# Wider token groups in a fused attention, FFN and expert kernel: 384 tokens for 256, and both halves of a pair's output in one go

## The chip, the cores and the metric

One core of one Trainium2 chip. The metric is the device time of one execution in microseconds (us), as the median of several runs. The kernel is written in Bass: each of the five engines (PE the matmul engine, DVE, ACT, POOL, SP) has its own list of instructions in a fixed order, and engines wait for one another through counting semaphores.

## The reference

Three stages follow one another. A linear attention with decay (4 batches, 8 heads, 768 steps, head size 48) gives `x` of 3072 tokens by 384. A gated layer without a nonlinearity then computes `h = ((x @ w1) * (x @ w2)) @ w3 @ w_out`, with an inner width of 1024. At last a noisy top-2 routing sends each token to two of eight experts, each a pair of matrices 384 by 1024 and 1024 by 384 with a ReLU between, and adds the two weighted results:

```python
for t in range(S):
    cur = np.einsum('bhd,bhe->bhde', u[None] * kt, vt)
    y[:, :, t] = np.einsum('bhd,bhde->bhe', rt, state + cur)
    state = wt[:, :, :, None] * state + np.einsum('bhd,bhe->bhde', kt, vt)
...
h = a * b @ w3
return (h @ w_out).astype(np.float32)
...
noisy_logits = logits + noise_scale * noise
top2 = np.argpartition(-noisy_logits, 2, axis=1)[:, :2]
...
h = np.maximum(x[mask] @ w1[e], 0.0)
out[mask] += top2_w[mask, k, None] * (h @ w2[e])
```

## The kernel before, in words

Every product is made from three matmuls of rounded parts (high by high, high by low, low by high), in a float type that PE runs at one column a cycle.

The program has three parts in time. **First part** (to about 107 us): the attention of batch 0, and beside it `w3 @ w_out` with the gate columns folded in (`wah`, `wal`, 400 columns wide), and the split of `w1` and `w2` into parts (`w12h`, `w12l`). **Middle part**: for batches 0 to 2, the gated layer works through the tokens of batch b in groups of TG = 256 (NG = 3 groups a batch) while the attention of batch b+1 is threaded between, pair of heads by pair of heads (HP = 4 pairs). **Finale**: the groups of batch 3 alone, then 31 visits of experts (4 early, 27 late), each of which gathers 256 or 128 token rows, multiplies them by an expert's matrices and adds the result into `result`.

A group runs through these steps. `turn`: ACT and DVE split the group's tokens, which SP has loaded from DRAM into a buffer (`xr`, three of them), into `xh` and `xl`. `up`: for each of eight blocks f of the inner width PE makes a and b side by side in one bank of PSUM (`pe_up`, line 807, 18 matmuls of 256 columns), ACT copies a out (`act_up`, L852), DVE multiplies it by b (`dve_up`, L885), ACT rounds the product (L848), DVE takes the rest (L878). Two banks alternate, so block f waits until block f-2 is multiplied. `down`: for each 128 tokens (ST = 2 tiles) 24 matmuls of 400 columns (`pe_down`, L823) into `fx` or bank 1; ACT copies the sum to `x2s` (L863), and SP stores 384 of its columns to DRAM (`sp_group_store`, L787). `route`: some twenty small operations of DVE and three of ACT choose two experts for each token. `place`: PE makes running counts (L836, L838), DVE turns them into slots, and POOL scatters one 8-byte entry for each token and choice into the table `slot_entry` in DRAM (`pool_scatter`, L985): one indirect DMA of 128 entries for each tile and choice, 4 for a group. `place` of a group comes in the `down` of the next one, after its first tile. `dve_place` waits at L967 until all scatters before its own have landed.

In the attention each pair of heads has steps too: `in` (transposes, L162), `score` (L177, into `pp`), `keys` (L186), `state` (L198), `scale`, and `out`: `pe_output` (L217 and L223) sums the output of half a batch's steps in the bank `yu`, ACT copies it to `yt` (L354), and the second half waits for that copy before it goes into the same bank.

The order on each engine comes from lists: `group_steps` gives the steps of a batch's groups, `pair_slots` those of the attention, and `threaded` deals the first over ten slots a pair in proportion to LENGTH. For the finale a loop adds the experts' steps by hand. There `split` n casts the n-th of seven pieces of an expert's weights (ACT, L1303, which waits for `piece_loaded`) and takes the rest (DVE, L1308); `tokens` transposes gathered rows (PE, L1199).

SP issues nearly all loads and stores in one order of its own and waits in it. For the first expert visit it waits until the scatters of batches 0 to 2 have landed (L1080), reads the expert's number, loads `who` (L1090) and then the seven pieces (L1100, L1104). POOL gathers rows for a visit (L1117), and the gather of visit 2 stands behind the scatters of the last group in POOL's order.

```python
elif kind == "down" and q == 1 and 1 <= n <= 4:
    finale.append(("split", 0, n - 1))
elif kind == "up" and q == 2 and n in (1, 3, 5):
    finale.append(("split", 0, 4 + n // 2))
elif kind == "down" and q == 2:
    finale.append(("tokens", 0, 0) if n == 0 else ("split", 1, n - 1))
```

## Time and profile before

| | |
|---|---|
| median of 3 runs | 1050.72 us (1050.07 to 1050.78) |
| profiled execution, own time | 1052.72 us |
| its span | 1051.0 us |
| granted TensorE clock, mean of the span | 0.99 |
| busy: PE, weight load, DVE, ACT, POOL | 96%, 91%, 67%, 56%, 21% |
| chain that ended last | PE 86%, DMA 4%, DVE 3%, issue 2% |
| matmul instructions | 7769 |
| first part, middle part with finale's groups, visits | about 0 to 107.7, to 541.8, to 1051 us |

The page is one execution. Busy times of PE hold overlaps: one matmul's record lasts longer than the distance to the next. What a stream of matmuls costs is read from the chain of waits, where a piece gives the time and the number of instructions. Idle time in square brackets stands before an instruction, with what ended it. The clock column is 1.00 at 2.4 GHz and 0.50 at 1.2 GHz.

### The profile page before, as it was taken

The numbers are of one execution on the slowest core, as the hardware profiler recorded it, in microseconds if no ns is written. First come the engines' busy times: TensorE is split into PE (matmuls) and PEld (weight loads), VectorE is DVE, ScalarE is ACT, GpSimd is POOL, SyncE is SP. The second block draws the span as 40 slices with busy tenths as digits, with TensorE's granted clock in tenths as the row PEclk, the third lists the DMA queues.
The fourth block names the chain that finished last, engine by engine and source line by source line (L and its number), as shares of the span: only waits on it lengthen the run. The fifth ranks groups of instructions, "written<-read, shape, count | busy, mean of one in ns | idle before, by whom it ended". The sixth has DMA issues, their size and how long they took to land.

```text
span 1051.0 us, 20538 instructions
## 1 busy us (share of the span) xinstructions
PE 1012.4 (96%) x7769; PEld 952.1 (91%) x7769; DVE 705.0 (67%) x1339; ACT 584.8 (56%) x1126; POOL 218.3 (21%) x210
## 2 busy tenths in 40 slices
PE   6999999989999899999998999999999999999995
PEld 5666899978999899999997999999999999999995
DVE  5887768666788687735685667575765857576570
ACT  4666445536555456533563566575665756566471
POOL 0000000110110110111324232433333234333421
PEclk9999999998999999999999999999999999999998
DMA  9655332333343422130757879787888978788851
GB/s 258 151 155 154 77 80 67 72 89 75 77 93 83 109 55 50 43 73 31 242 129 111 260 202 298 210 256 222 247 251 217 299 210 249 243 227 267 226 158 16
DMA packets 190887, 166.42 MB, mean 158 GB/s; under 512 B 118258, under 2 KB 174452, under 8 KB 190788
## 3 DMA queue, kind: packets, MB, share of 16 engines
q1 hardware_dynamic: 177012, 144.76, 48.2%
q0 software_dynamic: 12976, 20.32, 9.7%
q8 instruction: 62, 1.02, 0.5%
q14 instruction: 37, 0.30, 0.1%
q10 hardware_dynamic: 800, 0.02, 0.0%
HBM read 141.21 MB, written 25.22 MB: 158 GB/s over the span
## 4 chain that ended last, share of the span: by engine, by line
PE 86%; DMA 4%; DVE 3%; issue 2%; another core or an unknown queue 1%; POOL 1%; ACT 1%; SPq 1%; POOLq 0%; DVEq 0%; ACTq 0%
PE bank L807 19%; PE bank L1220 17%; PE pp L1236 17%; PE fx L823 5%; PE bank L823 5%; PE tr L162 3%; PE yu L1279 3%; PE yu L223 2%; PE pp L177 2%; PE fx L699 2%; PE bank L699 2%; PE yu L217 2%; PE tr L1199 2%; DMA xr<-ffn_out,who 2%; PE yu L1261 1%
## 5 line engine op out<-in xcount | busy, mean ns | idle before, releaser
L807 PE MATMUL bank<-xh,w12h 128*128 128x256 f32 x576 | 168.0, 292 | 0.6 <-DVE xl L483 0.6
L807 PE MATMUL bank<-xl,w12h 128*128 128x256 f32 x576 | 163.6, 284 | 0.8 <-issue 0.7
L807 PE MATMUL bank<-xh,w12l 128*128 128x256 f32 x576 | 163.5, 284 | 0.0
L1130 POOL DMA_INDIRECT result<-x2s,who x55 | 92.5, 1681 | 289.7 <-ACT x2s L1353 277.7
L1340 DVE SCALAR_TENSOR_TENSOR abl<-bank,abh 128x512 fp32r<-128x512 f32 x96 | 66.2, 690 | 111.7 <-ACT abh L1335 107.4
L985 POOL DMA_INDIRECT slot_entry<-entry,slot_i x48 | 48.5, 1010 | 381.1 <-DVE token_f L974 369.9
L807 PEld LDWEIGHTS bank<-xh,w12h 128*128 128x128 f32 x576 | 110.9, 193 | 3.3 <-issue 1.4
L807 PEld LDWEIGHTS bank<-xh,w12l 128*128 128x128 f32 x576 | 110.9, 193 | 1.0 <-issue 1.0
L807 PEld LDWEIGHTS bank<-xl,w12h 128*128 128x128 f32 x576 | 111.1, 193 | 0.0
L1220 PE MATMUL bank<-xh,set_up_h 128*128 128x256 f32 x384 | 109.2, 284 | 0.0
L1220 PE MATMUL bank<-xh,set_up_l 128*128 128x256 f32 x384 | 108.6, 283 | 0.0
L1220 PE MATMUL bank<-xl,set_up_h 128*128 128x256 f32 x384 | 108.6, 283 | 0.0
L1335 ACT ACTIVATE abh<-bank 128x512 fp32r<-128x512 f32 x96 | 57.5, 599 | 86.6 <-PE bank L1220 78.9
L885 DVE TENSOR_TENSOR ab_all<-a_sb,bank 128x256 f32<-128x256 f32 x96 | 40.2, 419 | 89.3 <-ACT a_sb L852 78.3
L1236 PE MATMUL pp<-set_down_h,abh 128*128 128x384 f32 x256 | 87.7, 343 | 0.0
L1236 PE MATMUL pp<-set_down_h,abl 128*128 128x384 f32 x256 | 85.7, 335 | 0.0
L1236 PE MATMUL pp<-set_down_l,abh 128*128 128x384 f32 x256 | 85.6, 334 | 0.0
L1117 POOL DMA_INDIRECT xr<-ffn_out,who x55 | 73.1, 1329 | 49.7 <-issue 25.9
L258 DVE RECIPROCAL kdiv<-decay 128x256 f32<-128x256 f32 x48 | 83.0, 1739 | 0.2
L852 ACT COPY a_sb<-bank 128x256 f32<-128x256 f32 x96 | 35.3, 368 | 85.6 <-PE bank L807 76.1
L1353 ACT ACTIVATE x2s<-pp,who 128x384 f32<-128x384 f32 x48 | 28.0, 582 | 84.8 <-PE pp L1236 79.8
L1220 PEld LDWEIGHTS bank<-xh,set_up_h 128*128 128x128 f32 x384 | 73.5, 191 | 0.5 <-DVE abl L1340 0.2
(249 smaller groups left out, 2752.1 us busy)
## 6 DMA issues: line engine op xcount, KB each, us to landing
up_raw<-in_moe_w SPq DMA_DIRECT2D x93, 512.0 KB
down_raw<-in_moe_w SPq DMA_DIRECT2D x124, 384.0 KB
padded<-in_w SPq DMA_DIRECT2D x32, 144.0 KB, 2.8
padded<-in_k SPq DMA_DIRECT2D x32, 144.0 KB, 2.8
padded<-in_r SPq DMA_DIRECT2D x32, 144.0 KB, 2.9
vs<-in_v SPq DMA_DIRECT2D x32, 144.0 KB, 2.9
attention_out<-yt SPq DMA_DIRECT2D x64, 72.0 KB, 1.9
xr<-attention_out SPq DMA_DIRECT2D x12, 384.0 KB, 3.4
```

Of the source, the lines that this page charges most:

```text
L258: nc.vector.reciprocal(kdiv[q % 2][:, :].rearrange("p (c x) -> p c x", c=NC)[:, two, :], decay[q % 2][:, two, 1:C + 1]).then_inc(inverse_r ...
L699: last = nc.tensor.matmul(sums[q % 2][:, 0:WA], w3T[q % 2][:, m, :], wo[:, m, :], start=(m == 0), stop=(m == KF - 1))
L807: last = nc.tensor.matmul(bank[f % 2][:, m * TG:(m + 1) * TG], wp[:, m, kk, f * P:(f + 1) * P], xp[:, kk, :], start=(n == 0), stop=(n == 3 ...
L823: last = nc.tensor.matmul(sum_at[s][:, 0:WA], xp[:, f, s * P:(s + 1) * P], wp[:, f, :], start=(f == 0 and n == 0), stop=(f == KF - 1 and n ...
L885: nc.vector.tensor_tensor(ab[f % 4], a_sb[f % 2][:, :], bank[f % 2][:, TG:2 * TG], ALU.mult).then_inc(ab_free, 1)
L985: nc.gpsimd.indirect_dma_start(slot_entry, bass.IndirectOffsetOnAxis(slot_i[:, s, n:n + 1], 0), entry[:, s, n, :], None).then_inc(scattere ...
L1117: nc.gpsimd.indirect_dma_start(xg[v % 2][:, s, :], None, stored, bass.IndirectOffsetOnAxis(who[v % 4][:, s, 0:1], 0)).then_inc(gathered[v ...
L1130: nc.gpsimd.indirect_dma_start(out, bass.IndirectOffsetOnAxis(who[v % 4][:, s, 0:1], 0), yo[v % 2][:, s, 0:DM], None, bounds_check=N - 1, ...
L1220: last = nc.tensor.matmul(bank[m % 2][:, f * T2:(f + 1) * T2], wp[:, kk, c:c + P], xp[:, kk, :], start=(n == 0), stop=(n == 3 * KD - 1))
L1236: last = nc.tensor.matmul(pp[:, s, 0:DM], xp[:, f, s * P:(s + 1) * P], wp[:, f, :], start=(f == 0 and n == 0), stop=(f == KF - 1 and n == 2))
L1335: nc.scalar.activation(hh[:, 2 * m:2 * m + 2, :].rearrange("p a t -> p (a t)"), bank[m % 2][:, :], ACT.Relu).then_inc(hh_ready, 1)
L1340: nc.vector.scalar_tensor_tensor(hl[:, 2 * m:2 * m + 2, :].rearrange("p a t -> p (a t)"), bank[m % 2][:, :], 0.0, hh[:, 2 * m:2 * m + 2, : ...
```

## The change

TG goes from 256 to 384, so a batch has NG = 2 groups and each group ST = 3 tiles. One block of a or b of 384 columns no longer shares a bank with the other: `up` has 16 steps a group (block f, then m = 0 for a and m = 1 for b), each 9 matmuls of 384 columns, in the three banks `bank[0]`, `bank[1]`, `fx` in turn (`half_bank`). Step n waits for what freed its bank: ACT's copy of a, or DVE's product, of step n-3. The tiles of `down` are summed in bank 1, `fx`, bank 1. A scatter of a group has six indirect DMAs, not four.

To find the memory, the three token buffers become one (`turned_in`, which is loaded again only when the tokens before it are turned), the three `x2s` one (ACT waits at the next `down` for its store), the four product buffers three, and some tables lie in other buffers' memory.

`pe_output`: the state's part of all six chunks is summed first, then the scores' part of half 0, then of half 1, half 0 in `yu` and half 1 in the first bank of `pp`; both `out` steps stand in one slot. PE no longer waits for ACT's copy of half 0, and the next pair's scores wait for both copies.

In the finale, `split` of visit 0 starts in the `up` of the last group (group 1) at its step 4, every second step, and `split` of visit 1 in its `down` from part 3. `store` of the finale's first group moves behind the first visit's loads on SP.

```diff
-TG = 256
+TG = 384
+HALVES = 2
...
-LENGTH = {"up": 8, "down": 6, "turn": 0, "route": 0, "place": 0,
+LENGTH = {"up": 6, "down": 6, "turn": 0, "route": 0, "place": 0,
...
+        def output_bank(half):
+
+            return (yu[:, 0:S // 2], pp[:, 0, 0:S // 2])[half]
+
         def pe_output(pe, b, q, half):
+
             g = HP * b + q
             if half == 0:
-                pe.wait_ge(state_ready, (NC - 1) * g + 2)
-                pe.wait_ge(att_ready, 2 * g + 1)
                 pe.wait_ge(yu_free, g + 1)
-            else:
                 pe.wait_ge(att_ready, 2 * g + 2)
                 pe.wait_ge(state_ready, (NC - 1) * (g + 1))
-                pe.wait_ge(y_ready, 2 * g + 1)
...
-                     [("out", q, 0), ("derive", q + 1, 1)],
-                     [("out", q, 1), ("in", q + 1, 2), ("derive", q + 1, 2)],
+                     [("out", q, 0), ("out", q, 1), ("derive", q + 1, 1)],
+                     [("in", q + 1, 2), ("derive", q + 1, 2)],
...
-                if q < 2:
-                    sp.wait_ge(y_stored[q], 32 * HP * (b + 1))
-                if not (isinstance(b, int) and b == 0):
-                    sp.wait_ge(turn_free, 2 * (NG * (b - 1) + q) + 2)
-                sp.dma_start(tokens_of(q), xa[:, bass.ds(b * S + q * TG, TG)].rearrange("(k p) t -> p k t", p=P)
+                sp.wait_ge(y_stored[q], 32 * HP * (b + 1))
+                need(sp, turn_free, 2 * (NG * b + q))
+                sp.dma_start(turned_in, xa[:, bass.ds(b * S + q * TG, TG)].rearrange("(k p) t -> p k t", p=P)
...
+                elif n >= 3:
+                    pe.wait_ge((a_ready, ab_free)[(n - 3) % HALVES], KF * i + (n - 3) // HALVES + 1)
+                p = 0
+                for kk in range(KD):
+                    for wp, xp in ((w12h, xh), (w12h, xl), (w12l, xh)):
+                        last = nc.tensor.matmul(half_bank[n % 3][:, 0:TG], wp[:, m, kk, f * P:(f + 1) * P], xp[:, kk, :],
+                                                start=(p == 0), stop=(p == 3 * KD - 1))
+                        p += 1
+                last.then_inc((a_full, b_full)[m], 1)
...
-                elif kind == "down" and q == 1 and 1 <= n <= 4:
-                    finale.append(("split", 0, n - 1))
-                elif kind == "up" and q == 2 and n in (1, 3, 5):
-                    finale.append(("split", 0, 4 + n // 2))
-                elif kind == "down" and q == 2:
-                    finale.append(("tokens", 0, 0) if n == 0 else ("split", 1, n - 1))
+                elif kind == "up" and q == 1 and n >= 4 and n % 2 == 0:
+                    finale.append(("split", 0, n // 2 - 2))
+                elif kind == "down" and q == 1:
+                    if n == 0:
+                        finale.append(("split", 0, 6))
+                    elif n == 1:
+                        finale.append(("tokens", 0, 0))
+                    elif 3 <= n < 8:
+                        finale.append(("split", 1, n - 3))
...
-                sp_group_store(sp, B - 1, 0)
                 sp_rows(sp, 0)
                 sp_weights(sp, 0)
                 for v in range(1, EARLY):
                     sp_rows(sp, v)
+                sp_group_store(sp, B - 1, 0)
+                sp_weights(sp, 1)
                 sp_group_store(sp, B - 1, 1)
-                sp_weights(sp, 1)
-                sp_group_store(sp, B - 1, 2)
```

ACT in the finale, before, around the first weight piece of visit 0 (`a_sb` holds a, `ab_all` the products, `set_up_h` and `up_raw` the expert's weights): it stands behind all eight blocks of the second group, in that group's `down`.

```order
L874 ACT_TABLE_LOAD
L874 ACTIVATE exp_gap<-gap 128x2 [waits gap_ready]
L852 COPY a_sb<-bank 128x256 [waits ab_full]
L848 CAST abh<-ab_all 128x256 [waits ab_free] x2
L477 CAST xh<-xr 128x512 [waits xr_loaded2,ab_full,x2_stored1]
L1303 CAST set_up_h<-up_raw 128x1024 [waits piece_loaded0]
L477 CAST xh<-xr 128x256 [waits ab_full]
L863 COPY x2s<-fx 128x400 [waits fx_full]
L1303 CAST set_up_h<-up_raw 128x1024 [waits piece_loaded1]
```

ACT at the same piece after the change (`work` holds both a and the products). It stands behind the copies of blocks 0 to 2 of group 1 and ahead of those of blocks 3 to 7.

```order
L858 COPY work<-fx 128x384 [waits a_full]
L852 CAST abh<-work 128x384 [waits ab_free,sum_full]
L858 COPY work<-bank 128x384 [waits a_full]
L852 CAST abh<-work 128x384 [waits ab_free]
L1321 CAST set_up_h<-up_raw 128x1024 [waits piece_loaded0]
L878 ACTIVATE exp_z<-x2s 128x24 [waits sum_free]
L880 ACT_TABLE_LOAD
L880 ACTIVATE ln_z<-one_z 128x24 [waits route_step]
L858 COPY work<-bank 128x384 [waits a_full]
L852 CAST abh<-work 128x384 [waits ab_free]
L1321 CAST set_up_h<-up_raw 128x1024 [waits piece_loaded1]
```

What moved: the wait for `piece_loaded0` now has the copies of five blocks and the roundings of six of the same group behind it on ACT.

DVE at the same place after the change: the product of block 2 (`work<-work,fx`), which frees the bank for step 8 of PE, follows the rest of the first piece and the first four operations of `route`.

```order
L897 TENSOR_TENSOR work<-work,bank 128x384 [waits abl_ready,b_full,a_ready] x2
L887 TENSOR_TENSOR abl<-work,abh 128x384 [waits abh_ready]
L1326 TENSOR_TENSOR set_up_l<-up_raw,set_up_h 128x1024 [waits w_high]
L924 TENSOR_SCALAR one_z<-exp_z 128x24 [waits exp_ready]
L925 SCALAR_TENSOR_TENSOR rest<-one_z,exp_z 128x24 [waits route_step]
L927 RECIPROCAL noisy<-one_z 128x24 [waits route_step]
L928 TENSOR_TENSOR rest<-rest,noisy 128x24 [waits route_step]
L897 TENSOR_TENSOR work<-work,fx 128x384 [waits b_full,abl_ready,a_ready,route_step]
L887 TENSOR_TENSOR abl<-work,abh 128x384 [waits abh_ready]
L1326 TENSOR_TENSOR set_up_l<-up_raw,set_up_h 128x1024 [waits w_high]
L897 TENSOR_TENSOR work<-work,bank 128x384 [waits abl_ready,b_full,a_ready]
```

What moved: before, DVE had no weight piece until the group's last product was made.

## Rows read from the trace of the kernel before

**Rows 1.** The page, part 4: the chain that ended last, by engine.

```profile
PE 86%; DMA 4%; DVE 3%; issue 2%; another core or an unknown queue 1%; POOL 1%; ACT 1%; SPq 1%; POOLq 0%; DVEq 0%; ACTq 0%
```

**Rows 2.** Chain of waits (start us, us, what), finale and routed stage.

```profile
460.87 17.27 PE bank L807 x144
...
652.33 4.17 PE yu L1279 x24
```

**Rows 3.** PE, one group by line (busy, mean ns | idle before, releaser).

```profile
L217 PE MATMUL yu<-rdec,state 48*64 48x128 f32 x320 | 24.8, 282 | 0.7 <-ACT yt L354 0.7
```

**Rows 4.** Chain of waits, the two placing matmul pairs at 340 us.

```profile
340.60 0.13 PE bank L836 x2
...
340.73 0.22 PE bank L838 x2
```

**Rows 5.** Timeline, PE and ACT (start us, us, engine, line, ... [idle before <-releaser]).

```profile
237.75 0.80 ACT L232 COPY wt<-tr 128x768 f32<-128x768 f32 x1 [7.50 <-remote]
...
238.69 1.09 PE L162 MATMUL tr<-ident,padded 128*128 128x128 f32 x4 [6.36 <-ACT wt L232]
...
358.73 0.74 PE L162 MATMUL tr<-ident,padded 128*128 128x128 f32 x5 [2.85 <-ACT wt L232]
```

**Rows 6.** Windows: us, busy of PE, PEld, DVE, ACT, POOL, PEclk, DMA, GB/s.

```profile
232.00:238.00 6.00, 0.33 (x3) 0.13 (x2) 0.00 (x0) 0.25 (x1) 0.00 (x0) 0.71 0.00 0
...
238.00:244.00 6.00, 5.31 (x26) 5.11 (x26) 3.34 (x12) 4.65 (x12) 0.00 (x0) 0.50 0.75 148
...
244.00:250.00 6.00, 6.00 (x66) 5.13 (x66) 4.45 (x7) 1.99 (x6) 0.00 (x0) 0.94 0.28 90
```

**Rows 7.** Timeline, POOL; then the landing of the group stores (line 787).

```profile
225.54 0.97 POOL L985 DMA_INDIRECT slot_entry<-entry,slot_i  x1 [0.30 <-issue]
...
DMA to landing us min/median/max: 3.5/8.4/9.7
```

**Rows 8.** Timeline of the finale's first group: PE, POOL, SP queue.

```profile
482.36 0.29 PE L836 MATMUL bank<-chosen,causal 128*128 128x16 f32 x2
...
484.89 0.97 POOL L985 DMA_INDIRECT slot_entry<-entry,slot_i  x1 [21.69 <-DVE token_f L974]
...
499.05 0.38 SPq L1090 DMA_DIRECT2D who<-slot_entry  x1
...
500.56 2.23 SPq L1100 DMA_DIRECT2D up_raw<-in_moe_w  x3
```

**Rows 9.** Timeline, ACT and DVE, first weight piece; DVE's multiply.

```profile
505.86 0.42 DVE L885 TENSOR_TENSOR ab_all<-a_sb,bank 128x256 f32<-128x256 f32 x1 [0.89 <-ACT a_sb L852]
...
507.21 1.04 ACT L1303 CAST set_up_h<-up_raw 128x1024 fp32r<-128x1024 f32 x1
...
508.28 1.23 DVE L1308 TENSOR_TENSOR set_up_l<-up_raw,set_up_h 128x1024 fp32r<-128x1024 f32 x1 [0.26 <-ACT set_up_h L1303]
```

**Rows 10.** Timeline of the finale's last groups: PE, POOL, DVE; then the chain of waits.

```profile
537.01 0.29 PE L836 MATMUL bank<-chosen,causal 128*128 128x16 f32 x2
...
542.18 1.50 POOL L985 DMA_INDIRECT slot_entry<-entry,slot_i  x1 [19.53 <-DVE token_f L974]
...
559.24 0.17 DVE L967 CAST slot_i<-slot_f 128x4 int32<-128x4 f32 x1 [2.77 <-DMA slot_entry<-entry,slot_i]
...
560.50 0.97 POOL L985 DMA_INDIRECT slot_entry<-entry,slot_i  x1 [11.88 <-DVE token_f L974]
...
576.29 0.87 PE tr L1199 x6
```

**Rows 11.** Windows, the same columns as rows 6.

```profile
572.00:578.00 6.00, 5.34 (x30) 5.05 (x31) 4.25 (x5) 3.61 (x7) 1.98 (x2) 0.72 0.96 208
```

**Rows 12.** Timeline, SP queue at the end of a batch; then the chain of waits.

```profile
207.78 0.80 SPq L153 DMA_DIRECT2D attention_out<-yt  x2
...
211.52 0.38 SPq L775 DMA_DIRECT2D xr<-attention_out  x1
...
223.16 2.77 PE bank L807 x18
```

243 lines of the change are left out of this document (124 added, 119 removed).

## The prediction

> **What bounds the kernel now.** First the chain that ended last: PE has 86% of it, DMA, DVE and the rest a few per cent each [rows 1]. So the time is PE's own pace plus the places where PE stands still. The pace is read from the same chain, where a piece gives time and count. A group's `up` is 144 matmuls of 256 columns in 17.27 us, 119.9 ns each; a stream of 24 matmuls of 384 columns takes 4.17 us, 173.8 ns each [rows 2]. The 128 further columns cost 53.9 ns, which is 2.4 columns a ns, so each matmul carries 119.9 - 256/2.4 = 13.2 ns whatever its width. Second, the places where PE stands. In the middle part the two largest are before the transposes at 238.69 (6.36 us) and at 358.73 (2.85 us), both behind an ACT copy `wt<-tr`; ACT itself had stood 7.50 us before that copy for something that isn't in the profile of this core's engines [rows 5]. The granted clock after the longer one is 0.50 for six microseconds and 0.94 for the next six, about 0.50 x 5.3 + 0.06 x 6 = 3.0 us of work lost [rows 6]. Third, the routing's scatters, since they stand ahead of everything in the finale. One starts at 484.89, 2.5 us after its group's `place`, and SP can read `who` only at 499.05, 14.2 us later [rows 8]; the next runs from 542.18 until DVE, waiting for it, passes L967 at 559.24, 17.1 us [rows 10]. Four indirect DMAs thus take 14 to 17 us, about 3.5 to 4.3 us each.
>
> **The change, part by part**, against the profiled execution (1052.7 us, 2.0 above the median of the runs; the sum below is moved by that at its end).
>
> *Wider `up`.* 12 x 144 = 1728 matmuls of 119.9 ns are 207.2 us; 8 x 144 = 1152 of 173.8 ns are 200.2 us: **-7.0**. All of it is PE's own, and PE is the chain, so it counts in full. DVE and ACT have the same elements in fewer operations and stay below PE. The columns of `down` are the same: nothing. The Trainium skill, page "TensorE: Matmul & The Clock Gate", section "Back-to-back issue gap", gives a lone matmul columns/2.4 + 2.5 ns. By that the saving would be 576 x 2.5 ns = 1.4 us, and the sum 5.6 higher, 1063 or 1064; rows 2, at 119.9 ns against its 109, speak for 13.2.
>
> *`place`.* Four groups fewer, each with a pair of 0.13 and 0.22 us [rows 4]: **-1.4**.
>
> *`out` in one go.* The wait of half 1 for ACT's copy is 0.7 us of idle time in all [rows 3]: **-0.7**. In exchange the next pair's scores wait for two copies. The lists put other steps between, so I count nothing; without them it is a copy of some half microsecond for each of 16 pairs, up to +5 if all were bare.
>
> *First `turn` of 384 tokens.* PE starts `up` after it; half as much again of an ACT and a DVE piece under 1.1 us: **+0.5**.
>
> *Loads at the end of a batch.* Tokens of group 0 are now loaded into the one buffer, 590 KB for 393 KB. Before, the store of y is issued at 207.78, the load at 211.52, and `up` begins at 223.16 [rows 12]. Transfers of 393 KB (the group stores, L787) land in 3.5 to 9.7 us, 9.7 where a scatter issued less than a microsecond before them is still under way [rows 7]. At half as much again, 5.3 plus 2.5 for the turn fits in the 11.6 us between load and `up`; 14.5 plus 2.5 would be 5.4 late, for three batches +16. A scatter must lie on each of them for that. Nothing, with +5 for one batch as upper case.
>
> *The scatter of six.* `place` is a third rarer, but a scatter has six indirect DMAs, in all 48 as before. One more pair of issues is +2.5 us at 1.27 us an issue; two more at 3.5 us are 7.0 if the transfers are what takes the time. I take 7.0, since the rest of the kernel sees the queues full for just that long [rows 8, 10].
>
> *The first visit's weights: the term that decides.* Let P be `place` of batch 2's last group, now in the finale's first `down`. Before: scatter at P + 2.5 (484.89), `who` at P + 16.7 (499.05), weights at P + 18.2 (500.56) [rows 8]; ACT's cast of the first piece ran at 507.21, behind the group's last roundings, with nothing to wait for [rows 9]. After: `who` at P + 16.7 + 7.0 = 23.7, weights 25.2, landed some 3.4 later (rows 7's fastest, for the same bandwidth) at 28.6, ACT's cast 1.04 and DVE's rest 1.23 [rows 9] to 30.9. Then DVE has four `route` operations, estimated 0.2 us each, and the product of block 2, 0.42 x 1.5 = 0.6 [rows 9]: P + 32.3. PE has 0.35 for `place`, a half `turn`'s wait of 0.5, two tiles of `down` (24 matmuls of 400 columns, 24 x (400/2.4 + 13.2) ns = 4.3 us each) and steps 0 to 7 of `up`, 9 x 173.8 ns = 1.564 each: P + 22.0. There it needs the bank that block 2's product frees. ACT's list has its wait for the first piece ahead of blocks 3 to 7, where before nothing but the turn stood behind it. So PE stands **10.3 us**, and after 6.36 us of standing the clock was at 0.50 [rows 5, 6], another 3.0: **+13.3**. Low end: the scatter's end doesn't depend on how many DMAs it has, 3.3 us; with the issue spacing alone, 5.8. I add no clock loss to these, being nearer to the short gap of rows 5 than to the long one. High end: 4.3 us for each further DMA and clock loss, 16.
>
> *The last groups.* Before: `place` 537.01, scatter 542.18, DVE passes L967 at 559.24, scatter of the last group 560.50, and behind it on POOL the gather of visit 2, whose rows PE transposes at 576.29, 39.3 us after that `place` [rows 10]; the clock there is 0.72 [rows 11], some 1.7 us lost. After: scatter at P + 2.5 (the shorter delay of rows 8, since DVE has no weights ahead of it), its end at 2.5 + 17.1 + 7.0 = 26.6, next scatter 27.9, tokens at 27.9 + 15.8 + 7.0 = 50.7. The work of PE between the same two points grows by the longer last group, one tile's `down`: 39.3 + 4.3 = 43.6. Later by 7.1, with more clock loss, estimated 1.3: **+8.4**. Low end: 2.5 in place of 7.0 twice, so 41.7 and -1.9.
>
> *Standstills of the middle part.* 6.4 + 2.9 + 3.0 of clock = 12.3 us hang on where a scatter meets ACT's waits for something outside the engines, in two of nine groups [rows 5, 6]; a scatter begins 225.54, ACT stands from 230 on [rows 7]. With six groups there, each scatter longer, and all moved, I take half: **-6**, between -12.3 and 0. The Trainium skill, page "DMA: Bandwidth & Descriptors", has each DMA engine take turns between queues a packet at a time; the 9.7 us landings beside a scatter agree. By it a longer scatter gives more such meetings, the end at 0.
>
> **Sum.** -7.0 - 1.4 - 0.7 + 0.5 + 13.3 + 8.4 - 6 = +7.1: 1052.7 + 7.1 = 1059.8, on the median **1058 us**.
>
> **Rivals.** *(a) The scatter doesn't grow* (faster). If 14 us is latency of a chain and not transfer, only the issues grow, the terms are +5.8 and -1.9, and with the middle standstills all gone (-12.3) the sum is -8.6 + 5.8 - 1.9 - 12.3 = -17.0, 1034; with half of them, 1040. For it: 1.27 us of issue a DMA is only 5 of the 14. Against: SP's and DVE's waits end 14 and 17 us after, long beyond one landing. *(b) The first visit's stall alone* (faster): the second is hidden, because visit 0 and 1 have work of PE to pull ahead, and the middle ones are gone: -8.6 + 13.3 - 12.3 = -7.6, 1043. *(c) The middle keeps its standstills or gets new ones* from the late load: 1058 + 6 = 1064, with one batch 5 us late 1069. For it: one buffer in place of three, which leaves no slack of a whole group. *(d) Matmuls of `up` cost by the column* (1.5 x 119.9 ns = 179.9): the 24 of rows 2 belong to another stage and might be better fed. No 7.0, 1065. *(e) The stall in the last group is taken back later*, since visits could run from work already done: PE is the chain, and all its work is still to be done, so a stall is only taken back where PE would have stood anyhow; it is in (b).
>
> **Chances.** Forecast 0.46 (1050 to 1064, the likeliest case's own range), (a) 0.20, (b) 0.10, (c) 0.17, (d) 0.07. The range has the upper part of (a)'s (1036 up), (b), (d) and (c) to 1068: 1036 to 1068. 0.2% is 2.1 us, about what a measurement of this kernel tells from no change. Faster, under 1048.6: (a), (b) and 0.01 of the forecast, 0.31. Same: 0.06, from the forecast's low end. Slower: the rest, 0.63.
>
> **What would show it.** In the new profile: pieces of the chain at L812 x144 of 25.0 us; transposes after `out` without idle time behind ACT `yt`; SP's wait for the first scatter in the finale of 16 us or more after the scatter's start; ACT waiting for the first weight piece and PE idle about 10 us at step 8 of the last `up`, with the clock at 0.50 behind it; DVE at L981 waiting for the scatter before; gather of visit 2 late by 7 us. **What makes it wrong**: first a six-DMA scatter that ends 14 us after its start, then (a) holds; a gap before step 8 under 3 us; middle-part gaps that sum to more than 12 us.

## The result and the profile after

Forecast 1058 us against 1050.72, measured 1056.78 (1056.38 to 1057.64, 4 runs) against 1050.39 for the kernel before in the same set: 1.0062 times as long, 95% interval 1.0043 to 1.0081. The change was run in two more sets: 0.9992 (0.9967 to 1.0016) and 1.0043 (1.0024 to 1.0062). So by its medians it is slower by up to 0.6%, in one set of three not at all; why that varies stays open. Its profiled execution took 1056.58 us, span 1054.9, for 1052.72 and 1051.0 of before: 3.9 us of difference, where the medians have 6.4.

The page of the kernel after, parts 1 and 4. PE has fewer instructions (7177 for 7769) and 13.7 us less busy time, and yet the span is longer. The chain still belongs to PE, but the page follows it back only to 485 us of the span, so that its shares add up to 54% [compare rows 1].

```profile
PE 998.7 (95%) x7177; PEld 942.0 (89%) x7177; DVE 687.9 (65%) x1151; ACT 566.9 (54%) x1034; POOL 218.4 (21%) x210
...
PE 46%; DMA 3%; DVE 2%; POOL 1%; ACT 1%; issue 1%; SPq 0%; POOLq 0%; DVEq 0%; ACTq 0%
```

PE's waits in the kernel after (what it waited for: us in total, times, longest). The first two are the two standstills of the finale that were forecast; the third holds 5.3 us in three pieces of the middle part (2.99, 1.97 and a small one) and 1.0 of the first part; the fourth is new.

```profile
PE tr L1219 <- DMA tokens<-ffn_out,who: 11.3, 1, 11.3
...
PE fx L812 <- DVE work L897: 6.8, 2, 6.4
...
PE tr L166 <- ACT wt L236: 6.3, 4, 3.0
...
PE bank L812 <- DVE work L897: 5.4, 5, 1.1
```

The following table cuts each profiled execution at the starts of PE's first `up` matmul, of the finale's first, and of visit 0's first, up to the start of the last matmul; "output" is the time from the start of each matmul of `pe_output` to the next instruction's, summed. The kernels below it are the experiments.

| kernel | first part | middle | finale's groups | visits | output |
|---|---|---|---|---|---|
| before | 107.7 | 353.0 | 81.1 | 497.2 | 49.1 |
| after | 106.2 | 343.7 | 88.9 | 503.8 | 43.4 |
| after, second and third set | 106.1, 105.5 | 340.7, 340.4 | 87.9, 86.9 | 501.0, 503.1 | 43.2, 43.6 |
| casts later | 106.2 | 339.4 | 78.7 | 505.5 | 43.9 |
| gather earlier | 105.3 | 340.2 | 87.5 | 490.9 | 43.2 |
| both | 104.5 | 339.2 | 78.7 | 490.8 | 43.2 |
| both, `route` later | 105.1 | 331.6 | 78.6 | 493.3 | 43.2 |
| the same, output undone | 108.0 | 332.5 | 78.6 | 490.9 | 48.7 |
| output undone alone | 107.0 | 339.2 | 87.4 | 502.9 | 48.7 |
| a scatter of four | 105.1 | 342.9 | 82.0 | 503.0 | 43.2 |
| before, output in one go | 104.8 | 335.7 | 82.3 | 500.0 | 43.2 |
| before, gather earlier | 107.6 | 342.7 | 87.7 | 490.5 | 49.9 |
| before, output and gather | 104.1 | 335.8 | 80.9 | 490.3 | 43.2 |

When the finale begins the change is 10.8 us ahead; in the finale's groups it loses 7.8 and in the visits 6.6.

**The first standstill.** Timeline of the kernel after, PE, POOL, SP's queue, ACT and DVE around the first weight piece (start us, us, engine, line; in brackets idle time and releaser), to be read beside [rows 8, 9].

```profile
479.23 0.29 PE L842 MATMUL bank<-chosen,causal 128*128 128x24 f32 x2
...
481.80 0.96 POOL L999 DMA_INDIRECT slot_entry<-entry,slot_i  x1 [30.42 <-DVE token_f L988]
...
499.46 0.37 SPq L1107 DMA_DIRECT2D who<-slot_entry  x1
...
500.62 1.40 SPq L1117 DMA_DIRECT2D up_raw<-in_moe_w  x3
...
504.55 1.04 ACT L1321 CAST set_up_h<-up_raw 128x1024 fp32r<-128x1024 f32 x1 [6.39 <-DMA up_raw<-in_moe_w]
...
505.63 1.23 DVE L1326 TENSOR_TENSOR set_up_l<-up_raw,set_up_h 128x1024 fp32r<-128x1024 f32 x1 [8.84 <-ACT set_up_h L1321]
...
507.75 0.55 DVE L897 TENSOR_TENSOR work<-work,fx 128x384 f32<-128x384 f32 x1
...
508.36 0.69 PE L812 MATMUL fx<-xh,w12h 128*128 128x384 f32 x1 [6.44 <-DVE work L897]
```

From `place` at 479.23: scatter after 2.6 us, `who` after 20.2, weights 21.4, cast 25.3, DVE's rest 26.4, and PE goes on after 29.1, having stood 6.44 us. Before, `who` was read 16.7 us after its `place`. ACT stood 6.39 us before the cast, which is the wait that had nothing behind it before. Next the chain of waits, where the same nine matmuls take 3.26 us behind the standstill and 1.56 (173 ns each) once the clock is back, and the windows (columns as in [rows 6]), where it is 0.54 for six microseconds:

```profile
508.36 3.26 PE fx L812 x9
...
523.00 1.56 PE bank L812 x9
```

```profile
502.00:508.00 6.00, 0.00 (x0) 0.00 (x0) 2.23 (x6) 3.04 (x5) 1.84 (x2) 0.89 0.97 339
...
508.00:514.00 6.00, 5.64 (x19) 5.64 (x20) 3.42 (x6) 3.29 (x5) 0.00 (x0) 0.54 1.07 375
...
514.00:520.00 6.00, 5.87 (x34) 5.55 (x33) 4.91 (x14) 2.21 (x4) 2.08 (x2) 1.00 0.79 293
```

**The second standstill.** PE, POOL and DVE of the kernel after, from `place` of the finale's first group to the rows of visit 2 (compare [rows 10]), then the chain piece and the window behind it:

```profile
529.63 0.30 PE L842 MATMUL bank<-chosen,causal 128*128 128x24 f32 x2
...
532.88 1.50 POOL L999 DMA_INDIRECT slot_entry<-entry,slot_i  x1 [16.07 <-DVE token_f L988]
...
554.17 0.16 DVE L981 CAST slot_i<-slot_f 128x6 int32<-128x6 f32 x1
...
555.42 0.97 POOL L999 DMA_INDIRECT slot_entry<-entry,slot_i  x1 [14.20 <-DVE token_f L988]
...
565.04 1.78 POOL L1134 DMA_INDIRECT tokens<-ffn_out,who  x1 [0.30 <-issue]
...
578.80 1.54 PE L1219 MATMUL tr<-ident,tokens 128*128 128x128 f32 x6 [11.34 <-DMA tokens<-ffn_out,who]
```

```profile
565.04 13.72 DMA tokens<-ffn_out,who
```

```profile
572.00:578.00 6.00, 0.00 (x0) 0.00 (x0) 0.00 (x0) 0.00 (x0) 1.83 (x2) 0.50 0.78 215
```

The scatter starts 3.3 us after `place`, the last one 25.8 after, and PE has its rows after 49.2. DVE at L981 did not wait: the scatter before had landed. The second of the two gathers is issued behind the six DMAs and lands 13.7 us later; PE has its rows 23.4 us after the last scatter's start, for 15.8 before.

**A wait that I had not forecast.** Timeline of DVE and PE at 185 us. DVE comes out of `rdec` (L275) at 185.1, then has the seven operations of `route`'s second part, and only then the product at L897 that frees PE's bank. PE stands 1.08 us, and so once more in each of four other groups of the middle part, always before step 12.

```profile
184.22 0.95 DVE L275 TENSOR_TENSOR rdec<-rt,decay 128x768 f32<-128x768 f32 x1
...
187.18 0.55 DVE L897 TENSOR_TENSOR work<-work,bank 128x384 f32<-128x384 f32 x1
...
187.79 0.44 PE L812 MATMUL bank<-xh,w12h 128*128 128x384 f32 x1 [1.08 <-DVE work L897]
```

**What the output costs PE.** One pair of heads in the kernel before, its two halves (8 and 12 matmuls, then 12 and 12), each up to the next instruction, and one pair in the kernel before with output in one go and the gather earlier (an experiment below; L218 and L223 are its output).

```profile
205.71 0.65 PE L217 MATMUL yu<-rdec,state 48*64 48x128 f32 x8
...
207.10 0.38 PE L807 MATMUL bank<-xh,w12h 128*128 128x256 f32 x1
...
209.43 0.87 PE L217 MATMUL yu<-rdec,state 48*64 48x128 f32 x12
...
211.04 0.66 PE L162 MATMUL tr<-ident,padded 128*128 128x128 f32 x4
```

```profile
199.85 0.65 PE L218 MATMUL yu<-rdec,state 48*64 48x128 f32 x8
...
202.55 0.39 PE L807 MATMUL bank<-xh,w12h 128*128 128x256 f32 x1
```

The halves take 1.39 and 1.61 us, together 3.00, and in one go 2.70. Inside a run these matmuls start in twos, 109 ns from one two to the next. From the last of the state's matmuls to the first of the scores' it is 199 ns, and from the last of a run to what follows 203, where 102 is usual, and the first two of each kind need 160 for 109. A pair in halves has each of this twice and in one go once, 0.15 us a time at either place. These 0.30 us in 15 pairs are 4.5 of the 5.9 us between 49.1 and 43.2. One pair more (at 31 us) took 3.74 for 2.70, with the wait for ACT's copy in it [rows 3], and one of the halves (at 244 us) fell into the low clock of [rows 6], 1.75 for 1.39.

### The profile page after: what moved, and what is told of

It is laid out like the page before. It is cut to its first block, busy times and chain, and to the rows that moved or that the text cites. A ratio compares the mean times of both kernels' runs of the same rounds, so it can differ in the third digit from the quotient of the medians.

```text
span 1054.9 us, 18983 instructions
## 1 busy us (share of the span) xinstructions
PE 998.7 (95%) x7177; PEld 942.0 (89%) x7177; DVE 687.9 (65%) x1151; ACT 566.9 (54%) x1034; POOL 218.4 (21%) x210
## 4 chain that ended last, share of the span: by engine, by line
PE 46%; DMA 3%; DVE 2%; POOL 1%; ACT 1%; issue 1%; SPq 0%; POOLq 0%; DVEq 0%; ACTq 0%
PE pp L1254 18%; PE bank L1238 18%; PE yu L1297 3%; PE tr L1219 2%; PE yu L1279 1%; PE fx L1279 1%; DMA tokens<-ffn_out,who 1%; DMA slot_entry<-entry,slot_i 1%; PE bank L829 1%; POOL slot_entry L999 1%; PE tr L1288 1%; PE fx L812 0%; PE fx L829 0%; DMA up_raw<-in_moe_w 0%; DVE set_up_l L1326 0%
## 5 line engine op out<-in xcount | busy, mean ns | idle before, releaser
L999 POOL DMA_INDIRECT slot_entry<-entry,slot_i x48 | 50.7, 1056 | 378.5 <-DVE token_f L988 366.3
L812 PE MATMUL bank<-xh,w12h 128*128 128x384 f32 x264 | 93.3, 354 | 6.8 <-DVE work L897 5.4
L812 PE MATMUL bank<-xl,w12h 128*128 128x384 f32 x264 | 89.5, 339 | 1.6 <-issue 1.6
L812 PE MATMUL bank<-xh,w12l 128*128 128x384 f32 x264 | 89.6, 339 | 0.0
L1254 PE MATMUL pp<-set_down_h,abh 128*128 128x384 f32 x256 | 87.7, 343 | 0.0
L1134 POOL DMA_INDIRECT tokens<-ffn_out,who x55 | 70.6, 1284 | 47.6 <-issue 27.5
L1371 ACT ACTIVATE x2s<-pp,who 128x384 f32<-128x384 f32 x48 | 27.9, 582 | 85.6 <-PE pp L1254 80.3
L1238 PEld LDWEIGHTS bank<-xl,set_up_h 128*128 128x128 f32 x384 | 73.5, 192 | 0.3
L1238 PEld LDWEIGHTS bank<-xh,set_up_l 128*128 128x128 f32 x384 | 73.5, 192 | 0.0
L1326 DVE TENSOR_TENSOR set_up_l<-up_raw,set_up_h 128x1024 fp32r<-128x1024 f32 x48 | 57.6, 1224 | 17.2 <-ACT set_up_h L1321 17.2
L897 DVE TENSOR_TENSOR work<-work,bank 128x384 f32<-128x384 f32 x48 | 26.6, 554 | 58.6 <-issue 43.3
L317 ACT ACTIVATE att<-ident,diag 128x128 f32<-128x128 f32 x192 | 61.1, 394 | 0.0
```

Source lines behind the costliest of these rows:

```text
L317: last = nc.scalar.activation(att[:, j, h, c, :], ident[:, :], ACT.Copy, scale=diag[:, 3 * j + c, h:h + 1])
L812: last = nc.tensor.matmul(half_bank[n % 3][:, 0:TG], wp[:, m, kk, f * P:(f + 1) * P], xp[:, kk, :], start=(p == 0), stop=(p == 3 * KD - 1))
L999: nc.gpsimd.indirect_dma_start(slot_entry, bass.IndirectOffsetOnAxis(slot_i[:, s, n:n + 1], 0), entry[:, s, n, :], None).then_inc(scattere ...
L1134: nc.gpsimd.indirect_dma_start(xg[v % 2][:, s, :], None, stored, bass.IndirectOffsetOnAxis(who[v % 4][:, s, 0:1], 0)).then_inc(gathered[v ...
L1238: last = nc.tensor.matmul(bank[m % 2][:, f * T2:(f + 1) * T2], wp[:, kk, c:c + P], xp[:, kk, :], start=(n == 0), stop=(n == 3 * KD - 1))
L1254: last = nc.tensor.matmul(pp[:, s, 0:DM], xp[:, f, s * P:(s + 1) * P], wp[:, f, :], start=(f == 0 and n == 0), stop=(f == KF - 1 and n == 2))
```

## The experiments

**Casts of visit 0's pieces later.**

```diff
-                elif kind == "up" and q == 1 and n >= 4 and n % 2 == 0:
-                    finale.append(("split", 0, n // 2 - 2))
+                elif kind == "up" and q == 1 and n >= 9 and n % 2:
+                    finale.append(("split", 0, n // 2 - 4))
                 elif kind == "down" and q == 1:
-                    if n == 0:
-                        finale.append(("split", 0, 6))
-                    elif n == 1:
+                    if n < 3:
+                        finale.append(("split", 0, 4 + n))
+                    if n == 1:
                         finale.append(("tokens", 0, 0))
```

> The change, with the pieces of visit 0's weights cast five steps of `up` later (behind steps 9, 11, 13, 15 and in the first three parts of `down`). From the last group's `up` (489.24) to visit 0's first matmul (538.82) the change takes 49.6 us for 39.2 us of PE work: 25.0 of `up`, 13.2 of `down`, 1.0 of small ones. Theory (ACT's wait for the first piece, ahead of five blocks' copies, stops PE at step 8 and halves the clock behind it): the gap of 6.4 us at step 8 and the clock loss of 3.3 go, the stretch falls to 40 to 41 us, the whole to 1056.8 - 9 = 1048, between 1046.5 and 1050. Rival 1 (given back): the pieces are now ready so late that visit 0 or 1 waits for them, or the longer standstill before visit 2 grows by what was gained; then the stretch is short and the whole above 1053. Rival 2 (not the first piece but `route` ahead of the products on DVE keeps PE waiting): the gap stays, above 1054.

Measured 1042.35 us (1038.46 to 1044.92), the kernel before 1046.45 in this set, ratio 0.9955 (0.9936 to 0.9973). Against the change that is 0.4 to 1.1% less, 4 to 11 us, depending on which of its three ratios is taken; 9 was expected, and against the first set's it is 11. (Told by the ratio, the whole is 1045.7 us of the first set's time, a little below the 1046.5 to 1050 that was expected.) The trace is clearer than the medians: the finale's groups take 78.7 us for 86.9 to 88.9, that is 8 to 10 less, and from the last group's `up` to visit 0 it is 39.2 us for 49.6, where 40 to 41 was expected. ACT now casts the first piece with no idle time ahead of it, and the waits of PE have the second standstill left, at full size:

```profile
500.12 1.05 ACT L1321 CAST set_up_h<-up_raw 128x1024 fp32r<-128x1024 f32 x1
```

```profile
PE tr L1219 <- DMA tokens<-ffn_out,who: 12.9, 1, 12.9
```

So theory one stands, rival 2 falls. Of rival 1 there is a little: the visits take 505.5 us, 1.7 to 4.5 more than in the change.

**Gather of visit 2 earlier.**

```diff
                 for q in range(NG):
+                    if q == NG - 1:
+                        pool_gather(pool, 2)
                     pool_scatter(pool, B - 1, q)
                 for v in range(NV):
-                    if v + 2 < NV:
+                    if 0 < v < NV - 2:
                         pool_gather(pool, v + 2)
```

> The change, with the gather of visit 2 placed in POOL's order ahead of the scatters of the last group, not behind them. In the change PE stands 11.3 us before visit 2's transposes at 578.80, and the clock loses some 1 to 2 more. Theory (the gather is issued behind six scatter DMAs and queues behind their transfers): the gap goes, the whole to 1056.8 - 12.5 = 1044, between 1042.5 and 1046.5. Rival 1 (the second half of what holds visit 2 is its weights or the late tables, not its rows): the gap shrinks to that, 3 to 6 us, the whole 1048 to 1051. Rival 2 (the gather itself slows what stands beside it): no gain, above 1054.

Measured 1037.76 us (1035.47 to 1038.57), ratio 0.9912 (0.9897 to 0.9926): 0.8 to 1.5% under the change. The visits take 490.9 us, 10 to 13 less. POOL's order, and PE's transposes of visit 2 without idle time:

```profile
535.80 0.99 POOL L1134 DMA_INDIRECT tokens<-ffn_out,who  x1 [0.30 <-issue]
...
549.72 1.01 POOL L999 DMA_INDIRECT slot_entry<-entry,slot_i  x1 [11.13 <-DVE token_f L988]
...
561.56 0.82 PE L1219 MATMUL tr<-ident,tokens 128*128 128x128 f32 x6
```

The expected 12.5 us are met within the spread of the change's own ratios, 8 to 15 us (the whole, 1041.1 us of the first set's time by the ratio, is a little below the expected 1042.5 to 1046.5). Neither rival has a trace for it. PE needs the rows 26 us after their gather is issued, so the gather loses nothing by the scatter behind it.

**Both.** Its edit is the two above.

> Both edits together: the casts of visit 0's pieces later, the gather of visit 2 ahead of the last scatters. If the two standstills are independent, as the theory has it, the gains add: -9 and -12.5, so 1035 to 1037, below the kernel before by 13 to 15 us. If one only moves time into the other, the sum is less by that amount: 1040 or more.

Measured 1027.86 us (1027.14 to 1030.24), ratio 0.983 (0.9815 to 0.9845), 18.6 us below the kernel before where 13 to 15 were expected. Taken from 1052.9 (1.0062 x 1046.45) the single edits gave 10.6 and 15.2 us and the two together 25.1, so they would add. But the change itself was not run in this set, and with its second ratio (0.9992) they would be 3.3, 7.9 and 17.8. That they add is read from the table: with both, the finale's groups and the visits have the lengths that each edit gave alone (78.7, and 490.8 for 490.9), and nothing is given back.

**Output undone.** `pe_scores` and `pe_output` as before, copies from `yu`, and the slots `("out", q, 1)` back beside `("in", q + 1, 2)`.

> The change with only its other part undone: the halves of a pair's output are made one after the other in the same bank again, in their old slots. Groups stay 384 tokens wide. Theory (the part is worth the wait for ACT's copy, 0.7 us of idle time in the trace before, and the step of PE is else the same work): +0.7, the whole 1056.5 to 1059. Rival 1 (the wait was paid in places that the trace puts down to something else, since both copies now come together): +3 or more. Rival 2 (holding the scores' first bank delays the next pair): the undone kernel is faster than the change by 1 us or more.

Measured 1050.95 us (1048.65 to 1052.64), ratio 1.0041 (1.0025 to 1.0057). This lies within the change's own three ratios and tells nothing alone: against the first it is 2 us faster, as rival 2 would have it, against the second 5 slower. The trace has the output at 48.7 us of PE for 43.2 to 43.6, and yet its middle part is not longer than those of the same width with the output in one go (339.2 for 339.2 to 343.7). PE's waits in that part are the five for DVE's product and no others:

```profile
PE bank L816 <- DVE work L901: 5.4, 5, 1.1
```

With the output in one go, PE also stands before the transposes, behind ACT's copy to `wt`: at 341 to 346 us for 2.99, 2.17 and 1.96 us in the change's three executions, 2.08 with casts later, 1.68 with the gather earlier, 1.19 with both, 2.69 with the scatter of four, and at 399 to 406 us for 0.7 to 2.0 us in each of the seven. In six of them it also stands 0.7 to 1.9 us at 225 to 227 us. With `route` later as well there is one of 1.00 at 337 us, and 0.84 just before it. That is eight executions of eight with output in one go at this width, and none of two with it undone. In the kernel before with output in one go there is none either (two executions). So what ACT waits for meets this part of the change at this width; why, no run shows.

**The change a second time.**

> The change itself, unaltered, once more, so that the other kernels of this set are read against it on the same chip. By the earlier pair of medians 1.0062 times the kernel before; nothing else is expected by any theory.

Measured 1048.00 us (1042.22 to 1049.82, 12 runs) against 1048.07: ratio 0.9992. The earlier 1.0062 is outside its interval. The profiled execution took 1049.64 us. In PE's timeline the standstill before visit 2 is short here and in three pieces; the one at 504 us is 5.37 for 6.44.

```profile
559.81 0.39 PE L1238 MATMUL bank<-xh,w12h 128*128 128x256 f32 x1 [0.86 <-DVE abl L1358]
...
564.11 0.39 PE L1238 MATMUL bank<-xh,w12h 128*128 128x256 f32 x1 [1.88 <-DVE abl L1358]
...
571.08 1.33 PE L1219 MATMUL tr<-ident,tokens 128*128 128x128 f32 x5 [3.64 <-DMA tokens<-ffn_out,who]
```

**The kernel before with output in one go.** The output part of the diff, applied to groups of 256.

> The kernel before (groups of 256 tokens) with only the output part of the change: both halves of a pair's output in one go, the second in the scores' first bank. Theory: the 0.7 us of waits for ACT's copy go and nothing else moves, ratio to the kernel before 0.998 to 1.0005. Rival (holding the scores' bank costs something, for the change without this part came out some 2 us faster than the ratio of the change would have it on that chip): 1.001 to 1.003, with standstills before a pair's scores (line 181 or so of the kernel) or before transposes.

Measured 1036.92 us (1034.73 to 1041.75), ratio 0.9914 (0.9886 to 0.9943). Neither theory nor rival had a gain of 9 us. The table has two sources of gain: the output's matmuls take 43.2 us for 49.1 (5.9), and the middle part had none of the standstills of [rows 5] in this execution (12.3 with the clock); the visits took 2.8 more. The two traces differ by 16.2 us where the ratio gives 9, because the kernel before was profiled in the first set alone and its times vary. PE's idle times have only 0.7 of the 5.9 [rows 3]; the rest is in the distances between matmul starts, as shown above.

**The kernel before with the gather earlier.** The same POOL edit.

> The kernel before with the gather of visit 2 ahead of the last group's scatters. Its trace has 4.0 and 0.7 us of idle PE and some 1.7 us of clock loss there. Theory (the same place costs both kernels, the change more): a gain of 5 to 7 us, ratio 0.993 to 0.995, that is a little over a third of what the same edit gave in the change (15 us). Rival (in the change the gather's move gained so much for another reason, such as contention between the gather and the weights' loads): in the kernel before it gains as much as there, or under 2 us.

Measured 1040.41 us (1035.44 to 1043.07), ratio 0.9927 (0.9897 to 0.9957). The visits take 490.5 us for 497.2: 6.7, as expected, and the same length as in the change with this edit, so this place cost the change (10 to 13) one and a half times to twice what it cost before. The finale's groups took 6.6 more here, with one standstill of 3.80 us at 465.04 and 3.4 us of clock behind it, ahead of the edit's place, and the middle part had neither of the standstills of [rows 5]. Whether such gaps differ between executions or between programs is not shown, since each of these kernels was profiled once.

**Both edits and `route` later.** On top of the two, `ROUTE_AT = (4, 9, 11, 13)` for `(4, 8, 10, 12)`.

> The change with the casts of visit 0's pieces later and the gather of visit 2 earlier, and the second, third and fourth part of `route` one step of `up` later (behind steps 9, 11 and 13 and not 8, 10 and 12), so that DVE makes the product of block 4 before the seven operations of `route`'s second part. The trace of the change has five standstills of PE of 1.08 us each, all waiting for that product. Theory (DVE comes to that product late because of its order, not because it is too slow): the five go, 5.4 us less than with the two edits alone, whose ratio to the kernel before was 0.983: 0.978. Rival (DVE is full there: the standstills move to the next product): as before, 0.982 to 0.984.

Measured 1023.53 us (1019.94 to 1026.49), ratio 0.9781 (0.9746 to 0.9816): 24.5 us below the kernel before, as expected, and the fastest here by a little. The five waits of 5.4 us for L897 are gone and the middle part takes 331.6 us for 339.2. PE's longest waits that are left behind those for the first loads, of the first line one in the first part:

```profile
PE tr L166 <- ACT wt L236: 2.0, 2, 1.0
...
PE bank L1238 <- issue: 1.9, 1, 1.9
...
PE bank L812 <- issue: 0.8, 1, 0.8
```

**The change a third time.**

> The change, unaltered, a third time. Two sets gave 1.0062 and 0.9992 times the kernel before, and the two traces differ mainly in what PE stands before visit 2: 11.3 us in one piece against 6.4 in three. If that standstill is what varies, this trace has a ratio between 0.998 and 1.007 and its sum of standstills from 540 to 600 us goes with it; if the whole kernel varies (pace of PE, middle part), the two do not go together.

Measured 1049.89 us (1049.32 to 1052.48), ratio 1.0043. PE stood 10.2 us before visit 2's transposes. High ratios (1.0062, 1.0043) go with long standstills there (11.3 and 10.2 us), the low one with the 6.4 in pieces. But the profiled executions of the second and third set took 1049.64 and 1049.89 us, all but the same, and the two ratios differ because the kernel before was 1048.07 in the one and 1046.12 in the other. So the standstill does not explain the ratios, and what does stays open.

**A scatter of four.** In one scatter only.

```diff
-                for s in range(ST):
+                for s in range(ST - 1 if i == NG * (B - 1) - 1 else ST):
                     for n in range(2):
```

> The change, with four and not six indirect DMAs in one scatter alone, that of batch 2's last group, for which SP waits before it reads the first visit's rows. It leaves out the entries of one tile of 128 tokens. Theory (the longer scatter is a part of the first standstill, the larger one being the order of the casts): the read of `who` comes 3.5 us earlier behind the scatter's start (14.2 and not 17.7), the gap at step 8 of the last `up` falls from 5 to 6.4 us to 2 to 3, the clock stays higher, the whole 4 to 6 us below the unaltered change of this set. Rival (the scatter ends when a transfer's own latency is over, however many there are): `who` moves by the issue of two DMAs at most, 2.5 us, the gap by no more, the whole by 1 to 3 us.

Measured 1046.85 us (1042.69 to 1049.41), ratio 1.0009 (0.9992 to 1.0025), 0.3% or 3.0 us (medians) under the unaltered change of this set, at the upper edge of the rival's 1 to 3. In the trace:

```profile
480.01 0.97 POOL L999 DMA_INDIRECT slot_entry<-entry,slot_i  x1 [30.55 <-DVE token_f L988]
...
491.45 0.38 SPq L1107 DMA_DIRECT2D who<-slot_entry  x1
...
508.67 0.44 PE L812 MATMUL bank<-xh,w12h 128*128 128x384 f32 x1 [1.95 <-DVE work L897]
```

`who` comes 11.4 us after the scatter's start, for 15.9 in the change of this set (493.76 behind 477.91), 4.4 us earlier; PE stands 1.95 us for 4.30, and the finale's groups fall from 86.9 to 82.0, 4.9 us, since the clock stays at 1.00 here. So the scatter's length is part of that standstill. How much two DMAs cost is less clear than this pair makes it: over all profiled executions `who` follows a scatter of four after 11.4, 13.7, 14.2, 14.4 and 14.6 us, one of six after 15.6 to 17.7 in nine executions, 16.1 in the median. Between the medians lie 1.9 us, no more than the 2.5 of two issues, which is the rival's mechanism. Counted from the last DMA's issue it is 9.9 to 10.7 us behind four (7.6 in this run) and 9.2 to 11.3 behind six, the same. The middle part was 2.5 us longer in this execution, before the edit's place, which is why the whole shows less.

**The kernel before with output and gather.**

> The kernel before (groups of 256) with the output part of the change and the gather of visit 2 ahead of the last scatters. It asks what the width of 384 alone is worth, beside the kernel with three edits (0.978 of the kernel before), since neither has the standstills of the finale. Theory: `up` saves 7.0 us and `place` 1.4, so this kernel is 8 us slower than that: 0.984 to 0.987 of the kernel before (the sum of both edits alone, 0.9914 and 0.9927, gives 0.984). Rival (the standstills that the width brings in the middle part eat it): 0.980 or less.

Measured 1025.20 us (1024.20 to 1026.27), ratio 0.9801 (0.9778 to 0.9825). PE's waits behind the first part are gone but for crumbs, of which this is the largest:

```profile
PE fx L823 <- DVE abl L878: 0.8, 3, 0.3
```

Against the change with three edits (0.9781) the width of 384 is worth 0.2%, 2 us, and the two intervals overlap. The traces part it: 4.2 us less in the middle, 2.3 less in the finale's groups, 1.0 more in the first part, 3.0 more in the visits (one gap of 1.9 us among them). The rival is nearer than the 8 us of the theory, and its reason holds for a part: in the middle the wider kernel stands 2.5 us and loses 1.7 to the clock, the other stands 0.8; the visits took as much again. Set the idle time aside and the width's own worth comes out, since in four kernels no clock was lost in the middle part. With output in one go it is 335.8 less 0.8 us of waits for groups of 256 and 339.2 less 10.0 for 384 ("both"), 5.8 us; with output in halves 342.7 less 2.9 and 339.2 less 5.4, 6.0 us. The prediction has 6.3 for these three batches of four.

**Three edits, output undone.**

> The change with the three edits of order (casts later, gather earlier, `route` later) and its output part undone: halves one after the other. In the traces the output's matmuls hold PE 5.9 us less in all when made in one go (43.2 for 49.1), and I had forecast 0.7. Theory (the gain is PE's time at the change from one kind of matmul to another, once less for each pair): 5 to 7 us slower than with the three edits, ratio to the kernel before 0.983 to 0.985. Rival (what the output part gained in the kernel before, 0.9% of it, was mostly that the middle standstills did not come): 0.978 to 0.980, where they are absent anyway.

Measured 1023.75 us (1023.67 to 1026.20), ratio 0.9795 (0.9771 to 0.9819) for 0.9781 with the output in one go. The rival is right about the whole: no difference that can be told. The output's own 5.5 us are there (48.7 for 43.2), and with them the first part is 2.9 shorter; but the middle part as a whole is only 0.9 shorter and the visits are 2.4 longer. In the middle PE stands 2.5 us and loses 1.7 to the clock with the output in one go, and stands for nothing over 0.15 us with it undone: the standstills described under "Output undone" take back what the matmuls save. Nor is the width's worth one number: without the output part it is 0.9795 against 0.9927 for the kernel before with its gather moved, whose trace has the standstill of 3.80 us and a middle part 10 us longer. So what the output part is worth depends on what else stands: 9 us in the kernel before, nothing that can be told here.

## Why the prediction was right, and where its terms were off

The number held, and the sign in two sets of three; the likeliest case had 1050 to 1064. Term by term, from the table and the rows:

- **Wider `up`, -7.0.** Right in pace: 1.56 us for nine matmuls, 173 ns, and so rival (d) falls. The width alone gave 5.8 and 6.0 us in the middle part, as worked out under "The kernel before with output and gather", of 6.3 forecast there. The Trainium skill ("TensorE: Matmul & The Clock Gate", "Back-to-back issue gap") gives 2.5 ns beside the columns for a lone matmul; in these streams 119.9 and 173 ns bear out some 13 ns. But "DVE and ACT stay below PE" failed locally: five waits of 1.08 us at step 12, 5.4 us. The order of DVE was the cause, since `route` one step later removed them.
- **`place`, -1.4; `turn`, +0.5.** Small, and no run changes them alone; the wait before the first `up` grew from 0.60 to 1.25 us, +0.65.
- **`out`, -0.7.** Mis-sized. I read PE's idle time and took it for the whole cost. The output's share of PE went from 49.1 to 43.4 us, -5.7. The other 5 are not in a wait: most of them are the two places fewer in each pair where PE goes from one kind of matmul to another, 0.30 us a pair, as shown above. What I counted as nothing in exchange is there too: at this width the part brings the standstills described under "Output undone".
- **Loads at the batch's end, 0.** Right: no standstill there.
- **First standstill, +13.3.** The mechanism held link by link, and the experiment that moves the casts gives the stretch back. The mis-sized step is "two more at 3.5 us are 7.0": the scatter held `who` up by 17.7 us, 3.5 more than before, and over all executions by 1.9 more, less than its two further issues (2.5); so PE stood 6.44 us and not 10.3; the clock took another 3 as forecast. By the stage (88.9 with it, 78.7 without) it is 10.2, and 8.2 to 9.2 in the other two executions. The low end ("issues alone", 5.8) fits what PE stood, 6.44, but I gave it no clock loss, and 6.4 us of standing was the very length at which [rows 5, 6] show the drop. (The high end of 16 is a slip of addition: two DMAs at 4.3 and the clock give 14.9.)
- **Last groups, +8.4.** Visits 6.6 longer (3.8 and 5.9 in the other two). The total was close, one link was wrong: DVE never waited at L981. The scatter before was over sooner; the last scatter was issued at +25.8 for my +27.9, and the time was lost behind it, 23.4 us to the rows where I had 22.8. By that sum the end of the scatter before would have come at 24.1 us after its start; DVE passed L981 after 21.3.
- **Middle standstills, -6.** Wrong. All of PE's idle time in the middle part was 10.2 us before and 12.8 after, and the clock lost while PE worked 3.0 and 1.7, so standing cost 1.3 us more, not 6 less. The standstills behind ACT went from 9.2 us to 5.0 (2.99 and 1.97), but 1.6 at 227.03 and the 5.4 behind DVE came. What I called chance is partly the kernel's own, since the two behind ACT come at the same places in every execution of the change; the kernel before with its output changed or its gather moved had none of its two.

The sum against the trace: -1.5 in the first part, -9.3 in the middle, +7.8 and +6.6, so +3.6; mine had -12.5 for the first two, then +11.2 (13.3 less the width's part) and +8.4. The gains were too large by 1.7 us, the losses by 5.2. Under the -9.3 of the middle part two errors cancel: I had -6.3 for the width, -0.5 for the output and -6 for the standstills, and it was some 11 less of PE's own work (the width's 6, the output's 4 to 5) and 1.3 more of standing. The median's +6.4 stood closer to my +7.1 than the profiled execution's +3.9, and the three sets' range from -0.1 to +6.4 us says that this was in part luck. Rival (a) was right that a longer scatter costs little beyond its issues, and wrong in what that leads to: even so PE stands long enough for the clock to fall; (b) falls since the second standstill was not hidden; (c) falls on the loads, but its other half, that the middle keeps its standstills or gets new ones, is what happened. What stays open is why the transfer behind the last scatter lands after 10.9 us in one execution and 13.7 in another, and what stalls ACT in the middle part. A hint, not tested: in the kernel before, one 16 KB transfer of the queue that the page calls `instruction` took 4.8 us from 229.9 and one 5.3 us from 351.7, and in both ACT fell idle (at 230.3 and 353.8); most others of this queue take 1 to 2 us. But one of 5.4 us from 467.8 has no such idle time beside it.

## What to carry to other kernels

When a group grows, look first at what is sized by the group but ordered by the step: here the scatter's DMAs, the casts and `route` took their old places in a list whose steps had become longer, and three edits of order were worth 22 to 29 us, by which of the change's ratios is taken, where the width itself, set against the kernel before with its own two edits, was worth about 2 (6 in the middle part once PE's idle time is set aside). A cast or a gather belongs in an engine's order behind the work that others wait for, not at the first place where its data might be there. Two merged steps can save more than the wait between them, since PE then changes its kind of matmul less often, and they can bring waits of their own elsewhere: compare the idle time and the work of the stage, not the whole alone.

## What the runs showed of the hardware

- SP, waiting for a scatter of four or six indirect DMAs (128 entries of eight bytes each), read `who` 14.2 and 16.1 us after its start in the median of five and nine executions, and 9.2 to 11.3 us after the last DMA's issue in all but one, so the length is mostly not the number of DMAs. The second gather behind the last scatter landed after 10.9 to 13.7 us behind six of them (six executions), and after 9.4 and 9.8 behind four.
- After 6.44 us in which PE stood, the granted clock was 0.54 for six microseconds; after 2.99 us (345 to 351 in the change) 0.72, but after 2.85 (358 to 364 in the kernel before) 1.00; after 1.95 us (the scatter of four) it was 1.00.
- Matmuls of the output cost 5.5 to 5.9 us less in all (704 of them) when a pair's 44 come in one run and not in two, with only 0.7 us of that in waits. At a change of kind two starts lay 199 to 203 ns apart where 102 was usual.
- The kernel before itself varied between 1042.06 and 1055.37 us within one set. A difference of 0.3% needs the stages of the traces beside the medians.
